# The way back ahead of the state product, and chunk 5's first mask two steps earlier

## The reference

```
for t in range(S):
    cur = einsum('bhd,bhe->bhde', u * k[t], v[t])
    y[t] = einsum('bhd,bhde->bhe', r[t], state + cur)
    state = w * state + einsum('bhd,bhe->bhde', k[t], v[t])
```

## Time and profile before

| | us |
|---|---|
| median of 3 runs | 419.09 |
| profiled execution | 419.95 |
| its span, first to last instruction | 418.2 |
| PE busy in it | 407.2 |
| DVE busy | 243.7 |
| POOL busy | 231.4 |
| ACT busy | 188.4 |

### The profile page before, as it was taken

How to read it: one execution, slowest core, us unless ns; L and a number is a source line. 1 busy time by engine, 2 the same in 40 slices (tenths; PEclk the granted TensorE clock), 3 DMA queues, 4 the chain that set the end, 5 groups by cost and what they waited for, 6 DMA issues and landing times.

```text
span 418.2 us, 9128 instructions
## 1 busy us (share of the span) xinstructions
PE 407.2 (97%) x3537; PEld 392.0 (94%) x3537; DVE 243.7 (58%) x576; ACT 188.4 (45%) x409; POOL 231.4 (55%) x239
## 2 busy tenths in 40 slices
PE   8899999999999999999999999999999999999994
PEld 8798799998999999999999999999999999999994
DVE  7688754375567546754663477785636545364521
ACT  4786453323433343334333465453646445574420
POOL 3789856556765785578334335166083562826531
PEclk9999999999999999999999999999999999999998
DMA  7998998122230303020009001826473835739000
GB/s 248 403 394 345 312 371 291 28 89 64 94 118 0 135 23 119 2 86 19 3 1 346 15 0 39 303 96 209 160 297 91 351 133 228 273 108 354 5 33 28
DMA packets 18649, 64.97 MB, mean 155 GB/s; under 512 B 2203, under 2 KB 11717, under 8 KB 16432
## 3 DMA queue, kind: packets, MB, share of 16 engines
q1 hardware_dynamic: 16816, 59.68, 39.2%
q0 software_dynamic: 1792, 4.73, 3.0%
HBM read 51.98 MB, written 13.21 MB: 156 GB/s over the span
## 4 chain that ended last, share of the span: by engine, by line
PE 84%; DMA 5%; DVE 3%; POOL 3%; issue 2%; ACT 1%; SPq 0%; POOLq 0%; DVEq 0%
PE bank L1361 25%; PE bank L1363 24%; PE bank L1362 24%; DMA wd_raw<-win 3%; DMA xrow<-slots 2%; PE bank L1379 2%; POOL g_lo L709 1%; PE bank L1408 1%; PE bank L1448 1%; PE bank L1444 1%; PE bank L1682 1%; PE bank L1437 1%; PE bank L1440 1%; PE bank L1535 1%; PE bank L1717 1%
## 5 line engine op out<-in xcount | busy, mean ns | idle before, releaser
L709 POOL TENSOR_TENSOR g_lo<-elu,g_hi 128x256 fp32r<-128x256 f32 x95 | 73.3, 773 | 90.0 <-ACT g_hi L874 89.4
L1361 PE MATMUL bank<-xt,wd_hi 128*128 128x256 f32 x285 | 80.5, 282 | 2.3 <-DVE elu L1189 2.3
L1363 PE MATMUL bank<-xt,wd_lo 128*128 128x256 f32 x285 | 80.4, 282 | 0.0
L1362 PE MATMUL bank<-xt,wd_hi 128*128 128x256 f32 x285 | 80.3, 282 | 0.0
L865 ACT ACTIVATE elu<-elu 128x256 f32<-128x256 f32 x96 | 40.1, 418 | 77.8 <-DVE elu L1181 77.2
L1361 PE MATMUL bank<-wd_hi,g_hi 128*128 128x392 f32 (+1 forms) x192 | 67.4, 351 | 0.0
L1189 DVE SCALAR_TENSOR_TENSOR elu<-elu,bank 128x256 f32<-128x256 f32 x96 | 40.3, 419 | 43.5 <-ACT elu L865 43.4
L1363 PE MATMUL bank<-wd_hi,g_lo 128*128 128x392 f32 (+1 forms) x192 | 65.2, 339 | 0.0
L1362 PE MATMUL bank<-wd_lo,g_hi 128*128 128x392 f32 (+1 forms) x192 | 65.1, 339 | 0.0
L874 ACT CAST g_hi<-elu 128x256 fp32r<-128x256 f32 x96 | 39.0, 406 | 44.0 <-DVE elu L1189 44.0
L1361 PEld LDWEIGHTS bank<-xt,wd_hi 128*128 128x128 f32 x285 | 53.9, 189 | 2.9 <-DVE elu L1189 2.9
(11 more groups left out here) (220 smaller groups left out, 948.1 us busy)
## 6 DMA issues: line engine op xcount, KB each, us to landing
we_raw<-wexp SPq DMA_DIRECT2D x8, 1536.0 KB, 6.9
wd_raw<-wexp SPq DMA_DIRECT2D x8, 1536.0 KB, 7.2
rkt<-rkt SPq DMA_DIRECT2D x12, 512.0 KB, 5.8
nat<-nat SPq DMA_DIRECT2D x9, 672.0 KB, 4.6
xrow<-slots SPq DMA_DIRECT2D x16, 193.0 KB, 7.1
wd_raw<-win SPq DMA_DIRECT2D x4, 768.0 KB, 10.5
wd_raw<-wout SPq DMA_DIRECT2D x4, 768.0 KB, 10.9
wo_tr<-wouttr SPq DMA_DIRECT2D x1, 3072.0 KB, 18.1
```

What stands on the lines that cost most here:

```text
L709: nc.gpsimd.tensor_tensor(g_lo[:, f % 4, :], elu[:, f % 2, :], g_hi[:, f % 4, :].bitcast(F32), ALU.subtract).then_inc(s_glo, 1)
L1361: mm(dst, w_hi, x_hi, start=start, stop=False)
L1362: mm(dst, w_hi, x_lo, start=False, stop=False)
L1363: return mm(dst, w_lo, x_hi, start=False, stop=stop)
```

## The change

In every step where both fall due, PE now runs back before outer. What used the order follows it: ACT's copy of y (x_hi) waits for outer too, because outer writes the same bank, and SP's load of a later chunk's natural rows waits for the outer that reads the buffer. Separately, mask0 of chunk 5 moves in the plan from step 25 to step 23.

```
@@ plan
             if c == 5:
-                steps.update(mask0=b + 3, mask1=b + 4)
+                steps.update(mask0=b + 1, mask1=b + 4)
@@ load_nat
                 wait_if(sp, s_rku, c - 4)
                 wait_if(sp, s_y, c - 1)
-                if c in (2, 3):
-                    sp.wait_ge(s_u, c - 1)
+                sp.wait_ge(s_u, n_states(c - 1))
@@ x_hi
                 act.wait_ge(s_y, c + 1)
+                if c >= 2:
+                    act.wait_ge(s_u, n_states(c + 1))
                 wait_if(act, s_h, FT * (c // 2 - 1))
@@ the loop of the steps, on PE
                     if c == 2:
                         bonus_sums(2)
+                    c = chunk_for("back", n, f)
+                    if c is not None:
+                        back(c)
                     c = chunk_for("outer", n, f)
                     if c is not None and leaves_state(c):
                         outer(c)
-                    c = chunk_for("back", n, f)
-                    if c is not None:
-                        back(c)
```

## The result

The changed kernel takes 416.37 us (median of 4 runs, 416.16 to 416.61), the kernel before 419.22 beside it (418.79 to 419.66): a ratio of 0.9932, 95% interval 0.9915 to 0.9949. That is 2.85 us less. Forecast were 2.0 us less and 417.1 us; the time lies inside the range, but only 0.07 us above its lower end. The profiled execution took 416.61 us with a span of 414.9.

A forecast was written before the change was run, and what follows sets the result against it. PE was taken to bound the kernel, busy 407.2 of 418.2 us, so only its waits count. 1.0 (wait for keys) + 0 (order) + 1.0 (mask) = 2.0 us: 419.09 - 2.0 = 417.1 us, range 416.3 to 418.5.

The forecast's parts named there:

- What bounds the kernel: PE is busy 407.2 of the 418.2 us span; only its waits or its own work can move the time.
- Edit 1: Back ahead of outer on PE in eight meetings; removes the wait for POOL's keys in chunk 2's: gain 1.00 us.
- 0.6 us to spare: Chunk 2's meeting: back runs until 39.3, POOL's keys are ready by 38.68, so outer follows without idle time.
- What is late next: Next hidden block: POOL's 1.46 us idle at 45.33 keeps some 0.4 with PE 1.0 us earlier, hiding its work.
- The price of the order in the other meetings: Full product behind outer instead of back: -0.2 to +0.24 us per meeting, eight times -1.6 to +1.9; taken as 0.
- The added waits: ScalarE's copy of y and SP's load of natural rows now wait for outer too: cost 0, the copy's bounds 0 to 0.6 us.
- Edit 2: Chunk 5's mask0 from step 25 to 23: PE waits 0.47 us at step 27, starts step 28 1.0 us earlier.
- The plain count of DVE's work: Moving chunk 5's mask: 0.62 us goes and 0.32 comes on DVE, a gain of 0.3 us.
- the forecast's rival: Step 23: the cast wins against POOL's g_lo, the whole 1.47 us wait at step 28 goes: 416.6 us; chance 0.12.
- The other rivals: Mask worth little, 417.7 to 418.1 (0.17); wait passed on, 418.1 (0.06); exit price, 418.6 (0.09); slower (0.06).

The follow-up runs named there:

- e6: Changed kernel, but outer stays ahead of back in the meeting of chunk 2, back first in the seven later ones: 418.08 us, ratio 0.9967.
- e9: Kernel before with one number changed: POOL scales chunk 2's keys at step 6 instead of step 7, outer still ahead of back: 417.94 us, ratio 0.9965.
- e7: The kernel before again, unchanged, for a second profile: 419.32 us, ratio 1.0001.
- e5: Changed kernel, but back ahead of outer in the meeting of chunk 2 alone, outer first in the seven later ones: 416.78 us, ratio 0.9936.
- e2: Kernel before with only chunk 5's mask0 moved from step 25 to step 23, outer still ahead of back: 418.04 us, ratio 0.9969.
- e1: Changed kernel with chunk 5's mask0 put back at step 25, so only back ahead of outer in every meeting: 417.75 us, ratio 0.9963.
- e3: The changed kernel again, unchanged, second measurement: 416.78 us, ratio 0.9943 to the kernel before.
- e11: The changed kernel unchanged, third measurement: 416.61 us, ratio 0.9937 to the kernel before.
- e4: Changed kernel with chunk 5's mask0 still in step 23 but behind the shift (cast, maximum, subtraction), not ahead of it: 416.15 us, ratio 0.9930.

## Why the prediction was right, and where it was off

- **What bounds the kernel.** Right: PE's busy time stayed, its idle time fell.
- **Edit 1, the wait before outer of chunk 2.** The mechanism was right (e6 brings the wait back, e9 removes it by another way). Its size was wrong: I took 1.00 us and called it the most it could be; it is 1.46 in the profiles with the fast start, and 1.53 us of PE's time. This is the term of the sum that was mis-sized, and it is most of what was missing: 1.46 + 1.0 makes 2.5 us, measured 2.85, 2.42 and 2.51. The cause is what e7 shows: my one profile had a start 0.78 us slow, and there POOL's keys came only 0.33 us later, so the late PE waited less for them. The "0.6 us to spare" shrinks for the same reason, to 0.14: a little later, and the keys would have held outer in its new place too.
- **What is late next.** Right in the outcome: no new wait of PE between 40 and 60 us. The slack was overrated. Of POOL's idle time before that g_lo (1.46 us, 1.44 in e7) 0.4 us was to be left; in the changed kernel nothing is, it starts straight behind the keys of the next chunk, and PE still doesn't wait for it:

```profile
43.45 1.06 POOL L708 TENSOR_TENSOR g_lo<-elu,g_hi 128x256 fp32r<-128x256 f32 x1
```

- **The price of the order in the other meetings.** Taken at 0, bounds -1.6 to +1.9 us. Right, as far as the scatter tells: e5's ratio to before is 0.9936, the changed kernel's 0.9932, 0.9943 and 0.9937. The gap of 0.20 us stays with the exit of back, whoever comes behind. That agrees with the drain of which the Trainium skill tells (TensorEngine Tiling (Array Packing), Key Properties), but not every change of shape shows such a gap here.
- **The added waits** of ScalarE and of SP's load: they weren't tried alone, but e6 differs from e2 only by them and by the order in seven meetings, and gained 1.24 us against 1.16; e1, with them, gained 1.45, and e9, without, 1.38.
- **Edit 2.** Right step by step, in the mechanism and in the sizes (1.0 us forecast, 1.16 in e2, 1.11 in the traces). PE's lead over the first profile was 1.91 us ahead of step 27; with that taken off, forecast and seen are: cast 0.75 us long and 0.74; min of step 24 late by 0.8 and 0.81 (84.85 against 85.95 - 1.91); min of step 25 late by 0.6 and 0.60; the product of step 27 late by 0.47 and 0.47; gates 0.95 us and 0.94; step 28 earlier by 1.0 in all and 1.06. What the Trainium skill says under SBUF — State Buffer, Who interferes with whom (an exclusive lock, taken by who issues first) agrees with each of these ends. The plain count of DVE's work, which gave 0.3, would have been wrong by 0.8 to 0.9 us.
- **Rivals.** The cast was issued 0.02 us behind g_lo, the margin that the forecast had found, and lost; in the other profiles with the mask at that place (e2, e3, e5, e6, e11) it is 0.02 to 0.03 us too, and the cast takes 0.74 us in each. The forecast itself couldn't be sure of so small a margin, so that it had the right side is partly luck. e4, which frees the cast by another order, shows what that is worth, 0.56 us; the forecast's rival had 0.47. The other rivals did not come about.

The remaining 0.3 us of the first pair of profiles lies in the experts, at one token tile's transposes, which wait for the gathered rows. The idle time of the weight load ahead of them is 0.42 us in the first profile of before, 0.67 in e7 and 0.17 in the changed kernel: it differs by 0.25 us between profiles of the same code, so the gain there isn't shown to be the change's. Why the first profile of before started slowly is open; no experiment addressed it.

The version that beats both kernels is the changed one with chunk 5's mask0 behind the shift: 415.88 us beside 416.61 for the changed and 419.12 for the kernel before.

## What to carry to other kernels

Where an engine waits for a result whose time is set by another chain, the wait's length depends on how early the engine came; take it from more than one profile, and don't call the idle time of one profile the most that can be gained. Where VectorE's queue holds small instructions beside GpSimd's long ones, don't add up an engine's work: write down which long instruction of the neighbour is in flight when each begins, and move the new work to where the short ones start ahead of it. Moving work within a step can be worth as much as moving it to another.

## What the hardware showed

- DVE's small instructions on two SBUF inputs, and its SBUF cast, last until the end of a POOL instruction issued as little as 0.02 us before them: 0.74 us instead of 0.16 for a cast of 8 elements. So do a tensor_scalar and a copy of 2 elements with one SBUF input, in the gates before; a reciprocal between them doesn't (POOL runs g_lo from 91.68 to 92.42 and its multiply from 92.38 to 93.39):

```profile
91.90 0.54 DVE L1129 TENSOR_SCALAR col<-col 128x2 f32<-128x2 f32 x1
92.48 0.17 DVE L1130 RECIPROCAL x2row<-col 128x2 f32<-128x2 f32 x1
92.56 0.85 DVE L1131 COPY x2row<-tokens 128x2 f32<-128x2 f32 x1
```

  The copy_predicated and the elu instructions, which read a PSUM bank, keep their 0.74 and 0.42 us beside POOL.
- A change of the weight shape on PE shows as 0.20 us of idle loading inside and behind back's products and as none behind outer's or scores', in either order.
- The idle time that the view of waits gives for PE is smaller than the delay of the product: 0.31 against 0.47 us at step 27, 0.57 for the product after it, and 1.46 against 1.53 before outer of chunk 2. The ends of matmuls are modelled in the profile; that this is the reason is not shown.
